# VectorE and ScalarE do the attention's operations between the two parts of an activation step in layer 1, not behind both (Trainium2, one core)

## The chip, the cores and the metric

The kernel runs on one core of a Trainium2 chip, in one launch. The metric is the device time of that launch in microseconds; the kernel before takes 1638.16 us in the median of 3 runs (1637.02 to 1641.31).

## What is computed

```python
a = exp(phi - max_s(phi)); a = a / (sum_s(a) + 1e-9)              # per (batch, head), softmax over the 576 rows
k_m = a^T k;  v_m = a^T v                                         # (32, 64) each: 32 memory slots per head
scores = q k_m^T / 8                                              # (576, 32)
attn = exp(scores - max_m(scores)); attn = attn / (sum_m + 1e-9)
x = attn v_m                                                      # heads side by side: x is (4608, 512)
h = x @ w1_in;  x = where(h > 0, h, exp(min(h, 0)) - 1) @ w1_out  # layer 1: 512 -> 2048 -> 512
h = x @ w2_in;  out = (h * clip(h + 3, 0, 6) / 6) @ w2_out        # layer 2, the same sizes
```

q, k, v and phi are (8, 8, 576, 64) and (8, 8, 576, 32), all float32.

## The kernel before, in words

**Tiling.** Layer 1 works on 16 units of 288 tokens (half a batch entry). A unit has 16 steps `f`, one for each 128 of the 2048 hidden features. In a step TensorE does `up1(f)`, six matmuls of 288 columns into a hidden bank of PSUM (L281 to L283, fed by `pT` and `w`), and `down1(f - 2)`, twelve matmuls that add an earlier step's features into the four accumulators (fed by `g_hi`, `g_lo`). Every product is made in three passes of high and low parts, so each activation leaves as a rounded copy `g_hi` and a rest `g_lo`.

**The step's activation** has five instructions on two engines, `step1`. First part: ScalarE's relu (L499) and exp (L501), then VectorE's combination `g` (L640), which is the last reader of the hidden bank and raises `turn_over`. Second part: ScalarE's copy `g_hi` (L503) and VectorE's `g_lo` (L642). `down1(f)` waits for `g_lo`.

**The attention** of group u + 2 (four heads) is done in the steps of unit u, for u = 0 to 13, as 11 stages; `STEP_OF` gives the step of each: row maximum of phi (S_PHI, step 0), its maximum over partitions (S_MAX, 1), subtraction and exp (S_SUB, 2), k_m and v_m (S_KV, 4), their transposes (S_KMT, 5), transposes of q (S_Q0 and S_Q1, 6 and 7), scores and their subtraction (S_SCORES, 9), exp (S_EXP, 10), sums and reciprocal on VectorE with the product on GpSimd (S_NORM, 11), transposes to `pT` (S_PT, 13). TensorE's instruction of a stage stands behind `up1(f)` and ahead of `down1(f - 2)`.

**Items.** x is never formed: v_m is multiplied into w1_in. That takes 8 items per batch entry: TensorE writes a hidden bank (L352), ScalarE copies `w_hi` (L481), VectorE makes `w_lo` (L633) and raises `turn_over`. Items stand in steps 6, 7, 9, 10, 12, 13 of odd units, 0 and 1 of even ones, and 0 to 3 of unit 0.

**Turns.** `up1` and items use two hidden banks in turn. The one that takes turn t waits until the turns up to t - 2 are over, so `up1` or an item waits for the L640 or L633 two turns back. TensorE's `half` gives the order: `up1(f)`, item, attention stage, `down1(f - 2)`. On ScalarE and VectorE each step was: `step1`, the copies of the last unit's accumulators (`leave`, step 1 only), item, attention stage. Every engine takes its instructions strictly as written, and each `wait_ge` holds all behind it. GpSimd (the product L724, the rests of w_out in unit 0) and SyncE (loads of the next group as soon as stages S_Q1, S_SCORES and S_PT of TensorE are done) are not touched. Layer 2 has no attention.

The few lines that count on VectorE:

```python
dve.wait_ge(e_made, t + 1)
nc.vector.scalar_tensor_tensor(g, g, -1.0, hid(at, HALF), ALU.add, ALU.max).then_inc(turn_over, 1)
dve.wait_ge(g_hi_made, t + 1)
nc.vector.tensor_tensor(g_lo, g, g_hi.bitcast(F32), ALU.subtract).then_inc(g_lo_made, 1)
```

Of the kernel before, what the change touches and what calls it, by code (L numbers as in the profile page):

```python
# [29 lines left out]
def build(nc, q, k, v, phi, w1_in, w1_out, w2_in, w2_out, out):  # L30
# [10 lines left out]
    DC, FC = D // P, F // P  # L41
# [11 lines left out]
    RING = 4  # L53
    AHEAD = 2
# [6 lines left out]
    with ExitStack() as ctx:  # L61
# [14 lines left out]
        def place(name, shape, dt, offset):  # L76
            return nc.alloc_sbuf_tensor_at(name, [P] + shape, dt, offset=base + offset)
# [11 lines left out]
        at = 4 * W  # L89
# [21 lines left out]
        def attention_set(tag, at_kvm, at_rows, at_kv, at_q, bank, stats):  # L111
            t = AttentionSet(bank)
            t.kvm = place("kvm" + tag, [3, P], F32, at_kvm)
            t.kmT = t.kvm[:, 2]
            t.row_max = t.kvm[0:ROWS, 2]
            t.rows = place("rows" + tag, [CH, P], F32, at_rows)


            t.kv = place("kv" + tag, [CH, MAC, KVW], F32, at_kv)
            t.qT = place("qT" + tag, [2, S], F32, at_kv)  # L120
            t.q = [place(f"q{i}" + tag, [CH, 2, DH], F32, x) for i, x in enumerate(at_q)]
            t.stats = stats
            t.phi_loaded, t.kv_loaded = sem("phi_loaded" + tag), sem("kv_loaded" + tag)
            t.q_loaded = [sem(f"q{i}_loaded" + tag) for i in range(2)]
            return t

        A = attention_set("", at, at + 3 * P * 4, a_kv, (a_q0, arena_bytes - Q_BYTES), ATT, small)
# [4 lines left out]
        g1 = [place(f"g1_{i}", [HALF], F32, at + i * ring1) for i in range(2)]  # L132
        g1_hi = place("g1_hi", [RING, HALF], F32R, at + 2 * ring1)
        g1_lo = place("g1_lo", [RING, HALF], F32R, at + (2 + RING) * ring1)
# [49 lines left out]
        def beyond(count):  # L184

            return not isinstance(count, int) or count > 0

        def hid(turn, n):
            return ps[:, HID + turn % 2, 0:n]
# [21 lines left out]
        def halves(a):  # L211
            return a[:].rearrange("p (b c) -> p b c", b=2)
# [4 lines left out]
        def kvm_block(t, h):  # L217
            parity = h % 2
            return t.kvm[h * M:(h + 1) * M, 0:2, parity * DH:(parity + 1) * DH]

        def nth(g, p):

            return 2 * p + g + 1 if isinstance(g, int) and g < AHEAD else 2 * g + p + 1
# [17 lines left out]
        def stages_at(f):  # L241
            return [stage for stage in STAGES if STEP_OF[stage] == f]
# [11 lines left out]
        def item_index(u, parity, n):  # L254
            return 4 * u + n + (NI // 2 if parity else 0)

        def first_turn(u, parity):

            if isinstance(u, int) and u == 0:
                return PRE  # L260
            return 20 * u + (4 if parity else 6)

        def turns(u, parity):

            at, found, made = 0, items_in(u, parity), []
            for f in range(FC):
                n = found.get(f)
                made.append((f, at, n))
                at += 1 if n is None else 2
            return made  # L270
# [181 lines left out]
        def _(act):  # L452
            def attention(g, stage, t, slot):
                if stage == S_SUB:
                    act.wait_ge(a_sub_made, g + 1)
                    nc.scalar.activation(t.rows_flat, t.rows_flat, ACT.Exp).then_inc(a_exp_made, 1)
                elif stage == S_KV:
                    act.wait_ge(a_inv_step, 2 * (g + 1))
                    for h in range(2):
                        rows = slice(h * M, (h + 1) * M)  # L460
                        op = nc.scalar.activation(kvm_block(t, h), t.ps_kv[rows],
                                                  ACT.Copy, scale=t.a_inv[rows])
                    op.then_inc(kv_copied_act, 1)
                elif stage == S_KMT:
                    act.wait_ge(kvT_done, g + 1)
                    nc.scalar.mul(t.kmT, t.ps_kmT, SCALE).then_inc(kmT_copied, 1)
                    nc.scalar.copy(vT[:, slot % 2], t.ps_vT).then_inc(vT_made, 1)
                elif stage in (S_Q0, S_Q1):
                    p = int(stage == S_Q1)
                    act.wait_ge(qT_done, nth(g, p))  # L470
                    nc.scalar.copy(t.qT[:, p, 0:HALF], t.ps_cols[:, 0]).then_inc(q_copied_act, 1)
                elif stage == S_EXP:
                    act.wait_ge(p_sub_step, 2 * (g + 1))
                    nc.scalar.activation(t.rows_flat, t.rows_flat, ACT.Exp).then_inc(p_exp_made, 1)
                elif stage == S_PT:
                    act.wait_ge(pT_done, g + 1)
                    nc.scalar.copy(halves(pT_hi[slot]), t.ps_cols).then_inc(pT_hi_made, 1)

            def item(i, n, at):
                act.wait_ge(item_done, i + 1)  # L480
                nc.scalar.copy(w1_hi[n // 2][:, n % 2], hid(at, BANK)).then_inc(w1_hi_made, 1)  # L481
# [12 lines left out]
            def step1(u, f, at, turn):  # L494
                t = u * FC + f
                if beyond(t - 1):
                    act.wait_ge(g_lo_made, t - 1)
                act.wait_ge(h_done, t + 1)
                nc.scalar.activation(g1[f % 2][:], hid(at, HALF), ACT.Relu, scale=-1.0).then_inc(r_made, 1)  # L499
                act.wait_ge(r_made, t + 1)  # L500
                nc.scalar.activation(g1[f % 2][:], g1[f % 2][:], ACT.Exp, scale=-1.0).then_inc(e_made, 1)  # L501
                act.wait_ge(turn_over, turn + 1)
                nc.scalar.copy(g1_hi[:, f % RING], g1[f % 2][:]).then_inc(g_hi_made, 1)  # L503

# [9 lines left out]
            def leave(u, dst):  # L514
                if beyond(u):
                    act.wait_ge(stored, 16 * u)
                for c in (0, 2):
                    act.wait_ge(acc_done, DC * u + c + 1)
                    nc.scalar.copy(dst[:, c], acc(c, dst.shape[2])).then_inc(acc_copied_act, 1)

            def half(u, um, attend):
                parity, first = um % 2, isinstance(u, int) and u == 0
                last = isinstance(u, int) and u == UNITS1 - 1
                for f, at, n in turns(u, parity):
                    step1(u, f, at, first_turn(u, parity) + at)
                    if f == LAG - 1 and not first:
                        leave(u - 1, y_sb)
                    if n is not None:
                        item(item_index(u, parity, n), n, at + 1)
                    if attend:  # L530
                        for stage in stages_at(f):
                            attention(u + AHEAD, stage, A, (um + AHEAD) % 4)
                    if first:
                        split_out_hi(f, 0)
                    if last:
                        split_in_hi(f)
                        if f >= 10:
                            split_out_hi(f - 10, 1)
# [40 lines left out]
        def _(dve):  # L579
# [55 lines left out]

            def step1(u, f, at):
                t = u * FC + f
                g, g_hi, g_lo = g1[f % 2][:], g1_hi[:, f % RING], g1_lo[:, f % RING]
                dve.wait_ge(e_made, t + 1)
                nc.vector.scalar_tensor_tensor(g, g, -1.0, hid(at, HALF), ALU.add, ALU.max).then_inc(turn_over, 1)  # L640
                dve.wait_ge(g_hi_made, t + 1)
                nc.vector.tensor_tensor(g_lo, g, g_hi.bitcast(F32), ALU.subtract).then_inc(g_lo_made, 1)  # L642

# [19 lines left out]
            def half(u, um, attend):  # L663
                parity, first = um % 2, isinstance(u, int) and u == 0
                for f, at, n in turns(u, parity):
                    step1(u, f, at)
                    if f == LAG - 1 and not first:
                        leave(u - 1, y_sb)
                    if n is not None:
                        item(item_index(u, parity, n), n, at + 1)  # L670
                    if attend:
                        for stage in stages_at(f):
                            attention(u + AHEAD, stage, A, (um + AHEAD) % 4)
                    if isinstance(u, int) and u == UNITS1 - 1 and f == FC // 2:
                        x2_round(0, 0)

# [219 lines left out]
```

## Time and profile before

| what | value |
|---|---|
| median of 3 runs | 1638.16 us (1637.02 to 1641.31) |
| the profiled execution: its own time / its span | 1637.58 us / 1635.8 us |
| mean granted TensorE clock | 0.997 of full speed |
| TensorE busy | 1579.6 us, 97% of the span |
| VectorE, ScalarE, GpSimd busy | 659.4, 654.2, 132.2 us |
| DMA | 79.50 MB, mean 49 GB/s |

The span is from the first to the last instruction; the execution's own time has 1.8 us around it. Matmul rows overlap: consecutive ones start about 0.13 us apart and each is shown for about 0.29 us. "[1.41 <-DVE kvm L583]" behind a row is the idle time of that engine before it and what ended it.

### The profile page before, as it was taken

What the parts mean: (1) busy time and instruction counts of PE and PEld (TensorE: products, weight loads), DVE (VectorE), ACT (ScalarE), POOL (GpSimd) and SP (SyncE); (2) the same over time, 40 slices, a digit from 0 to 9 for tenths busy, and PEclk for the clock granted to TensorE, in tenths of its full rate; (3) what the DMA queues carried; (4) which work ended last, traced back from release to release, by engine and by line L of the source; (5) the groups of instructions that cost most, each with busy time, mean ns of one, the idle gap of its engine ahead of it and who ended that gap; (6) DMA issues with size and microseconds to landing.
All of it is one profiled execution on the core that took longest, in us unless ns stands there. A gap on an engine that the chain in (4) does not pass through costs nothing.

```text
span 1635.8 us, 25445 instructions
## 1 busy us (share of the span) xinstructions
PE 1579.6 (97%) x9840; PEld 1364.1 (83%) x9840; DVE 659.4 (40%) x1163; ACT 654.2 (40%) x1363; POOL 132.2 (8%) x99
## 2 busy tenths in 40 slices
PE   4999999999999999999999999999999999999999
PEld 3788989879888798888998888888888888888887
DVE  4455555554555545555353232232323232323222
ACT  2565555545555455555573222222222222222222
POOL 0320000000000000000182101010101010101000
PEclk9899999999999999999999999999999999999999
DMA  9423221232212222120321010101010101010000
GB/s 246 136 42 66 52 59 42 47 68 52 59 38 52 64 55 59 38 52 17 143 79 65 0 52 0 52 0 51 0 51 0 51 0 51 0 49 2 7 19 26
DMA packets 178101, 79.50 MB, mean 49 GB/s; under 512 B 152400, under 2 KB 160592, under 8 KB 178000
## 3 DMA queue, kind: packets, MB, share of 16 engines
q1 hardware_dynamic: 168528, 76.07, 17.6%
q10 hardware_dynamic: 9472, 2.07, 0.8%
q8 instruction: 65, 1.06, 0.3%
q14 instruction: 36, 0.29, 0.1%
HBM read 59.24 MB, written 18.87 MB: 48 GB/s over the span
## 4 chain that ended last, share of the span: by engine, by line
PE 57%; issue 37%; DVE 2%; ACT 2%; POOL 1%; ACTq 1%; POOLq 0%; DVEq 0%
PE ps L281 18%; PE ps L283 18%; PE ps L282 18%; POOL rows L724 1%; PE ps L352 1%; DVE g L640 1%; PE ps L331 1%; ACT g_hi L503 0%; PE ps L302 0%; ACT g L501 0%; ACT g L499 0%; DVE g_lo L642 0%; ACTq L556 0%; PE ps L320 0%; ACTq L554 0%
## 5 line engine op out<-in xcount | busy, mean ns | idle before, releaser
L281 PE MATMUL ps<-g_hi,w_out_lo 128*128 128x288 f32 x1024 | 314.1, 307 | 0.9 <-POOL w_out_lo L713 0.6
L282 PE MATMUL ps<-g_lo,w_out_hi 128*128 128x288 f32 x1024 | 301.7, 295 | 0.0
L283 PE MATMUL ps<-g_hi,w_out_hi 128*128 128x288 f32 x1024 | 301.7, 295 | 0.0
L509 ACT ACTIVATE g<-ps,one_half 128x512 f32<-128x512 f32 x144 | 99.3, 690 | 465.6 <-PE ps L283 465.6
L648 DVE SCALAR_TENSOR_TENSOR g<-g,ps 128x512 f32<-128x512 f32 x144 | 99.2, 689 | 450.5 <-ACT g L509 450.5
L281 PE MATMUL ps<-x_hi,w_in_lo 128*128 128x512 f32 x576 | 224.1, 389 | 0.0
L283 PE MATMUL ps<-x_hi,w_in_hi 128*128 128x512 f32 x576 | 224.1, 389 | 0.0
L282 PE MATMUL ps<-x_lo,w_in_hi 128*128 128x512 f32 x576 | 224.1, 389 | 0.0
L281 PE MATMUL ps<-w_out_hi,g_lo 128*128 128x512 f32 x576 | 224.1, 389 | 0.0
L282 PE MATMUL ps<-w_out_lo,g_hi 128*128 128x512 f32 x576 | 224.1, 389 | 0.0
L283 PE MATMUL ps<-w_out_hi,g_hi 128*128 128x512 f32 x576 | 224.1, 389 | 0.0
L640 DVE SCALAR_TENSOR_TENSOR g<-g,ps 128x288 f32<-128x288 f32 x256 | 115.4, 451 | 256.8 <-ACT g L501 256.7
L281 PEld LDWEIGHTS ps<-g_hi,w_out_lo 128*128 128x128 f32 x1024 | 192.3, 188 | 23.2 <-issue 20.3
L282 PEld LDWEIGHTS ps<-g_lo,w_out_hi 128*128 128x128 f32 x1024 | 192.5, 188 | 0.1
L283 PEld LDWEIGHTS ps<-g_hi,w_out_hi 128*128 128x128 f32 x1024 | 192.2, 188 | 0.0
L642 DVE TENSOR_TENSOR g_lo<-g,g_hi 128x288 fp32r<-128x288 f32 x256 | 130.5, 510 | 127.8 <-ACT g_hi L503 127.8
L499 ACT ACTIVATE g<-ps 128x288 f32<-128x288 f32 x256 | 104.8, 409 | 179.6 <-PE ps L283 160.7
L503 ACT CAST g_hi<-g 128x288 fp32r<-128x288 f32 x256 | 110.8, 433 | 142.6 <-DVE g L640 142.6
L281 PE MATMUL ps<-pT_hi,w_lo 128*128 128x288 f32 x512 | 151.9, 297 | 4.6 <-issue 3.0
L282 PE MATMUL ps<-pT_lo,w_hi 128*128 128x288 f32 x512 | 151.4, 296 | 0.0
L283 PE MATMUL ps<-pT_hi,w_hi 128*128 128x288 f32 x512 | 151.1, 295 | 0.0
L650 DVE TENSOR_TENSOR g_lo<-g,g_hi 128x512 fp32r<-128x512 f32 x144 | 108.7, 755 | 99.0 <-ACT g_hi L512 99.0
(108 smaller groups left out, 1950.7 us busy)
## 6 DMA issues: line engine op xcount, KB each, us to landing
layer_out<-y_sb SPq DMA_DIRECT2D x16, 576.0 KB, 3.1
x_raw<-layer_out SPq DMA_DIRECT2D x9, 1024.0 KB, 6.9
kv<-in_k SPq DMA_DIRECT2D x60, 144.0 KB, 3.4
kv<-in_v SPq DMA_DIRECT2D x60, 144.0 KB, 3.5
q<-in_q SPq DMA_DIRECT2D x60, 144.0 KB, 2.9
w_in_raw<-in_moe_w_in SPq DMA_DIRECT2D x8, 1024.0 KB, 10.9
w_out_raw<-in_moe_w_out SPq DMA_DIRECT2D x8, 1024.0 KB, 6.2
out<-out_sb SPq DMA_DIRECT2D x8, 1024.0 KB, 5.1
```

The costliest lines, as they stand in the source:

```text
L281: nc.tensor.matmul(dst, a_lo, b_hi, start=first, stop=False)
L282: nc.tensor.matmul(dst, a_hi, b_lo, start=False, stop=False)
L283: return nc.tensor.matmul(dst, a_hi, b_hi, start=False, stop=last)
L331: mm = nc.tensor.matmul(chunk(t, j, P)[0:ROWS, lm], t.qT[:, p, j * ROWS:(j + 1) * ROWS], t.kmT[:, lm], start=True, stop=True)
L352: mm = nc.tensor.matmul(hid(at, BANK)[lm], vT[:, gi, lm], w_in_raw[:, 2 * gi + p, cols], start=True, stop=True)
L499: nc.scalar.activation(g1[f % 2][:], hid(at, HALF), ACT.Relu, scale=-1.0).then_inc(r_made, 1)
L503: nc.scalar.copy(g1_hi[:, f % RING], g1[f % 2][:]).then_inc(g_hi_made, 1)
L509: nc.scalar.activation(g2[f % 2][:], hid(f, BLOCK), ACT.Relu, bias=one_half[:, 0:1], scale=1.0 / 6.0).then_inc(e_made, 1)
L640: nc.vector.scalar_tensor_tensor(g, g, -1.0, hid(at, HALF), ALU.add, ALU.max).then_inc(turn_over, 1)
L642: nc.vector.tensor_tensor(g_lo, g, g_hi.bitcast(F32), ALU.subtract).then_inc(g_lo_made, 1)
L648: nc.vector.scalar_tensor_tensor(g, g, 1.0, hid(f, BLOCK), ALU.min, ALU.mult).then_inc(turn_over, 1)
L650: nc.vector.tensor_tensor(g_lo, g, g_hi.bitcast(F32), ALU.subtract).then_inc(g_lo_made, 1)
```

## The change

In each step of layer 1, ScalarE's and VectorE's part of the attention stage moves from behind the item to between the first part of the activation and the second. The instructions and waits are the same; TensorE's, GpSimd's and SyncE's programs are the same.

```diff
 # ScalarE, step1
                 nc.scalar.activation(g1[f % 2][:], g1[f % 2][:], ACT.Exp, scale=-1.0).then_inc(e_made, 1)
+
+            def step1_hi(u, f, turn):
+
+                t = u * FC + f
                 act.wait_ge(turn_over, turn + 1)
                 nc.scalar.copy(g1_hi[:, f % RING], g1[f % 2][:]).then_inc(g_hi_made, 1)
...
                     step1(u, f, at, first_turn(u, parity) + at)
+                    if attend:
+                        for stage in stages_at(f):
+                            attention(u + AHEAD, stage, A, (um + AHEAD) % 4)
+                    step1_hi(u, f, first_turn(u, parity) + at)
                     if f == LAG - 1 and not first:
                         leave(u - 1, y_sb)
                     if n is not None:
                         item(item_index(u, parity, n), n, at + 1)
-                    if attend:
-                        for stage in stages_at(f):
-                            attention(u + AHEAD, stage, A, (um + AHEAD) % 4)
...
 # VectorE, step1
                 nc.vector.scalar_tensor_tensor(g, g, -1.0, hid(at, HALF), ALU.add, ALU.max).then_inc(turn_over, 1)
+
+            def step1_lo(u, f):
+
+                t = u * FC + f
+                g, g_hi, g_lo = g1[f % 2][:], g1_hi[:, f % RING], g1_lo[:, f % RING]
                 dve.wait_ge(g_hi_made, t + 1)
                 nc.vector.tensor_tensor(g_lo, g, g_hi.bitcast(F32), ALU.subtract).then_inc(g_lo_made, 1)
...
                     step1(u, f, at)
+                    if attend:
+                        for stage in stages_at(f):
+                            attention(u + AHEAD, stage, A, (um + AHEAD) % 4)
+                    step1_lo(u, f)
                     if f == LAG - 1 and not first:
                         leave(u - 1, y_sb)
                     if n is not None:
                         item(item_index(u, parity, n), n, at + 1)
-                    if attend:
-                        for stage in stages_at(f):
-                            attention(u + AHEAD, stage, A, (um + AHEAD) % 4)
```

In the new file the lines of VectorE are five further on: L640 is L645, L642 is L652, L633 is L638, L583 is L588, L612 and L615 are L617 and L620.

VectorE, steps 0 and 1 of an odd unit (S_PHI is the reduction into `kvm`, S_MAX the one of `stats`). Before:

```order
L640 SCALAR_TENSOR_TENSOR g_0_80<-g_0_80,ps 128x288
L642 TENSOR_TENSOR g_lo<-g_0_80,g_hi 128x288
L583 TENSOR_REDUCE kvm<-rows 96x128
L640 SCALAR_TENSOR_TENSOR g_1_81<-g_1_81,ps 128x288
L642 TENSOR_TENSOR g_lo<-g_1_81,g_hi 128x288
L657 COPY y_sb<-ps 128x288 x2
L587 TENSOR_REDUCE stats<-ps 128x1
```

Now:

```order
L645 SCALAR_TENSOR_TENSOR g_0_80<-g_0_80,ps 128x288
L588 TENSOR_REDUCE kvm<-rows 96x128
L652 TENSOR_TENSOR g_lo<-g_0_80,g_hi 128x288
L645 SCALAR_TENSOR_TENSOR g_1_81<-g_1_81,ps 128x288
L592 TENSOR_REDUCE stats<-ps 128x1
L652 TENSOR_TENSOR g_lo<-g_1_81,g_hi 128x288
L667 COPY y_sb<-ps 128x288 x2
```

The two reductions moved ahead of `g_lo`, and the second also ahead of the accumulators' copies.

VectorE, steps 9 and 10 of an odd unit (S_SCORES and an item in step 9, an item in step 10). Before:

```order
L640 SCALAR_TENSOR_TENSOR g_1_81<-g_1_81,ps 128x288
L642 TENSOR_TENSOR g_lo<-g_1_81,g_hi 128x288
L633 TENSOR_TENSOR w_lo_61<-ps,w_hi_57 128x512
L612 TENSOR_REDUCE stats<-ps 96x24
L615 TENSOR_TENSOR rows<-ps,stats 96x768
L640 SCALAR_TENSOR_TENSOR g_0_80<-g_0_80,ps 128x288
```

Now:

```order
L645 SCALAR_TENSOR_TENSOR g_1_81<-g_1_81,ps 128x288
L617 TENSOR_REDUCE stats<-ps 96x24
L620 TENSOR_TENSOR rows<-ps,stats 96x768
L652 TENSOR_TENSOR g_lo<-g_1_81,g_hi 128x288
L638 TENSOR_TENSOR w_lo_61<-ps,w_hi_57 128x512
L645 SCALAR_TENSOR_TENSOR g_0_80<-g_0_80,ps 128x288
```

The item's `w_lo`, which ends a turn, now stands behind the stage's two operations and `g_lo`.

## Rows read from the trace of the kernel before

**Rows 1.** Busy time by engine (PE, PEld, DVE, ACT, POOL) in a stretch of layer 2.

```profile
1000.00:1600.00 600.00, 600.00 (x2649) 496.82 (x2648) 173.71 (x242) 151.74 (x235) 27.68 (x6) 1.00 0.07 23
```

**Rows 2.** Waits of TensorE over the span: us in total, times, longest.

```profile
PE ps L290 <- DVE kvm L583: 18.5, 9, 8.2
PE ps L337 <- POOL rows L724: 8.7, 8, 3.1
PE ps L352 <- DVE w_lo L633: 3.1, 8, 0.7
```

**Rows 3.** Timeline, odd unit, steps 0, 1 and 5: start us, us, instruction, idle before.

```profile
302.91 0.46 DVE L640 SCALAR_TENSOR_TENSOR g<-g,ps 128x288 f32<-128x288 f32 x1 [0.99 <-ACT g L501]
303.86 0.46 DVE L642 TENSOR_TENSOR g_lo<-g,g_hi 128x288 fp32r<-128x288 f32 x1 [0.50 <-ACT g_hi L503]
304.24 1.45 DVE L583 TENSOR_REDUCE kvm<-rows 96x128 f32<-96x768 f32 x1
...
305.74 0.30 PE L290 MATMUL ps<-ident,kvm 96*128 96x96 f32 x1 [1.41 <-DVE kvm L583]
...
215.76 0.14 PEld L308 LDWEIGHTS ps<-ident,kvm 128*128 128x128 f32 x1 [0.25 <-ACT kvm L461]
```

**Rows 4.** Timeline, even unit, steps 0 to 2, VectorE and TensorE.

```profile
254.53 0.45 DVE L640 SCALAR_TENSOR_TENSOR g<-g,ps 128x288 f32<-128x288 f32 x1 [0.97 <-ACT g L501]
...
256.57 1.50 DVE L583 TENSOR_REDUCE kvm<-rows 96x128 f32<-96x768 f32 x1
...
257.07 1.08 PE L352 MATMUL ps<-w_in_raw,vT 128*64 128x512 f32 x4
...
260.58 0.30 PE L283 MATMUL ps<-pT_hi,w_hi 128*128 128x288 f32 x1
261.55 0.35 PE L293 MATMUL ps<-ident,stats 128*96 128x128 f32 x1 [0.67 <-DVE stats L587]
```

**Rows 5.** Timeline, odd unit, items of steps 6, 7, 9 and 10.

```profile
322.91 0.69 DVE L633 TENSOR_TENSOR w_lo<-ps,w_hi 128x512 fp32r<-128x512 f32 x1
...
324.50 1.08 PE L352 MATMUL ps<-w_in_raw,vT 128*64 128x512 f32 x4
...
333.42 0.69 DVE L633 TENSOR_TENSOR w_lo<-ps,w_hi 128x512 fp32r<-128x512 f32 x1
334.26 0.95 DVE L612 TENSOR_REDUCE stats<-ps 96x24 f32<-96x768 f32 x1
335.24 0.95 DVE L615 TENSOR_TENSOR rows<-ps,stats 96x768 f32<-96x768 f32 x1
...
336.60 0.65 PE L352 MATMUL ps<-w_in_raw,vT 128*64 128x512 f32 x2
```

**Rows 6.** Timeline, steps 11 to 13 of an even unit, and the item of step 13 in an odd one.

```profile
292.34 0.39 DVE L640 SCALAR_TENSOR_TENSOR g<-g,ps 128x288 f32<-128x288 f32 x1
293.24 1.06 DVE L642 TENSOR_TENSOR g_lo<-g,g_hi 128x288 fp32r<-128x288 f32 x1 [0.50 <-ACT g_hi L503]
...
292.50 1.48 POOL L724 TENSOR_TENSOR rows<-rows,stats 96x768 f32<-96x768 f32 x1 [48.74 <-DVE stats L625]
...
294.04 0.38 PE L337 MATMUL ps<-ident,rows 96*128 96x96 f32 x2 [0.73 <-POOL rows L724]
...
346.57 0.65 PE L352 MATMUL ps<-w_in_raw,vT 128*64 128x512 f32 x2 [0.32 <-DVE w_lo L633]
```

**Rows 7.** Timeline, unit 0, steps 2 and 3: VectorE's subtraction, TensorE's item.

```profile
56.30 0.94 DVE L590 TENSOR_TENSOR rows<-rows,ps 96x768 f32<-96x768 f32 x1
...
57.56 0.65 PE L352 MATMUL ps<-w_in_raw,vT 128*64 128x512 f32 x2
```

**Rows 8.** Groups of ScalarE over the span: busy us, mean ns of one, idle before.

```profile
L503 ACT CAST g_hi<-g 128x288 fp32r<-128x288 f32 x256 | 110.8, 433 | 142.6 <-DVE g L640 142.6
L481 ACT CAST w_hi<-ps 128x512 fp32r<-128x512 f32 x64 | 37.1, 582 | 1.0 <-PE ps L352 0.9
L456 ACT ACTIVATE rows<-rows 96x768 f32<-96x768 f32 x15 | 12.7, 846 | 19.6 <-DVE rows L590 19.6
```

More of the change, by code:

```diff
@@ L637, in step1 @@
                 t = u * FC + f
-                g, g_hi, g_lo = g1[f % 2][:], g1_hi[:, f % RING], g1_lo[:, f % RING]
+                g = g1[f % 2][:]
                 dve.wait_ge(e_made, t + 1)
                 nc.vector.scalar_tensor_tensor(g, g, -1.0, hid(at, HALF), ALU.add, ALU.max).then_inc(turn_over, 1)
+            def step1_lo(u, f):
+                t = u * FC + f
+                g, g_hi, g_lo = g1[f % 2][:], g1_hi[:, f % RING], g1_lo[:, f % RING]
                 dve.wait_ge(g_hi_made, t + 1)
```

## The prediction, made before the changed kernel was run

> **What bounds the kernel now.** I read the busy time by stretch first. In layer 2 TensorE has no gap at all: 600.00 us busy in a stretch of 600.00 [rows 1]. So nothing on the other engines can be won there, and whatever TensorE gains or loses in layer 1 arrives whole at the end of the kernel. Then I read the waits of TensorE [rows 2]. They are short and belong to the attention: it waits for VectorE's row maximum at L290 (9 times; one of 8.2 us is in the start-up, 7 are the 1.41 us of the odd units), for GpSimd's product at L337, and for the `w_lo` of an item at L352. Each is a place where the attention's work is ready later than TensorE is. Last, the timeline of one even and one odd unit, step by step, because the change only reorders two engines inside a step: the question at each step is what stands in front now, what stands behind, and how long TensorE can do without it.
>
> The pattern that the change uses is in [rows 3]: VectorE finishes `g` at 303.37, then idles 0.50 us until ScalarE has copied `g_hi`, makes `g_lo` from 303.86, and only then starts the reduction at 304.24 (instructions without a wait start 0.08 us before the one ahead is shown ended). With the stage in between, its VectorE operation starts 0.95 us earlier (304.24 less 303.29) if its input is there, and part of it fills that idle time. In return `g_lo`, and behind it an item's `w_lo`, are later.
>
> **Odd units (1, 3, ... 13: seven).**
> - L290, step 1. The reduction ends at 303.29 + 1.45 = 304.74 and TensorE goes on 0.05 us later as before, at 304.79 for 305.74 [rows 3]. **-0.95 us**, all of it inside the wait of 1.41.
> - L308, step 5, waits 0.25 us for the copies of k_m and v_m [rows 3]; those copies also start about 1 us earlier against TensorE. **-0.2 us**.
> - Step 6. `w_lo` is now behind the copy of q: ScalarE's copy waits for TensorE's transposes, so I get `w_lo` ending at 324.16, for 323.60 before. The next item needs it at 324.50 [rows 5]. Hidden, with 0.34 us left of a cover of 0.90; if that cover fell short the price would be the rest.
> - Step 9, the expensive one. L612 cannot start earlier: it waits for TensorE's scores, at 334.26 either way. L612 and L615 end at 336.19; then come `g_lo` (336.11 to 336.57) and `w_lo` (336.59 to 337.28), which used to end at 334.11. The item of step 10 needs that bank at 336.60 [rows 5] and starts at 337.33. **+0.73 us**, a wait that does not exist now.
> - Step 11 to 13. The item of step 13 waits 0.32 us for `w_lo` [rows 6], because the `g_lo` ahead in the queue takes 1.06 us instead of 0.46 while GpSimd's L724 runs. In the new order the sums, the reciprocal and then `g_lo` of step 11 follow each other, and GpSimd's product is triggered earlier relative to TensorE, which step 10 has held back 0.73. I get this `w_lo` ready before TensorE comes: **-0.32 us**.
>
> Together -0.95 - 0.2 + 0.73 - 0.32 = -0.74, times 7: **-5.2 us**.
>
> **Even units (2, 4, ... 12: six).**
> - Step 0. The reduction runs from 254.90 to 256.40, `g_lo` to 256.78, `w_lo` to 257.49; the item of step 1 starts at 257.54 for 257.07 [rows 4]. **+0.47 us**.
> - Step 2. L293 waits 0.67 us for the maximum L587, which stands behind the copies of the accumulators and an item's `w_lo` [rows 4]. In the new order it stands ahead of them. TensorE could start L293 at 260.58 + 0.15 and, with the 0.47 from above, does at 261.20 for 261.55. **-0.82 us**, net of step 0 -0.35.
> - Steps 11 to 13. L724 is triggered 0.95 us earlier. The row says who comes first: the VectorE instruction behind the reciprocal starts at 292.34, GpSimd at 292.50 [rows 6], so the new follower `g_lo` is ahead of GpSimd by 0.16 us. That `g_lo` and L724 disturb each other is seen from the other side: `g_lo` takes 1.06, ending 0.32 after L724. If GpSimd waits for `g_lo`, it starts 0.38 later, at 291.93, ends at 293.41, and L337 starts at 293.47 for 294.04: **-0.57 us**. Without such a wait it would be up to the whole 0.73 idle. I take the first.
>
> The Trainium skill (SBUF — State Buffer, section "Who interferes with whom") says that a VectorE operation with two SBUF inputs and a GpSimd operation that reads SBUF exclude each other for a whole instruction, the first to start keeping the ports. The row with 1.06 us agrees with its half "the loser fully blocks"; no row shows VectorE starting first. By that rule the term is the one taken; by the other reading of the row, sharing without order, it would be up to -0.73 and the sum 1 us lower.
>
> Together -0.92, times 6: **-5.5 us**.
>
> **Unit 0** has items in steps 0 to 3 beside stages 0 to 2, and a loss. In step 2, `w_lo` moves from ahead of L590 (56.30) to behind L590 (0.94), ScalarE's exp (0.85), `g_hi` (0.43), `w_hi` (0.58) and its own 0.69 [rows 7, 8]. L590 itself starts about 1 us earlier, at some 55.5; the chain of 3.5 us ends near 59.0 where the item of step 3 started at 57.56: +1.5. A phi load that lands late in step 0 can add 1; the earlier product in step 11 gives back about 0.65. I take **+1.5 us**; bounds 0 and +2.5.
>
> **What else moves.** A later `g_lo` is needed by `down1` and by relu two steps on. The largest delay, in step 9, leaves it ready at 336.57, before even the item of step 10 begins, and its users are in step 11: nothing; without that cover it would cost what exceeds it. No stage waits for something of its own step that now stands behind it. SyncE's loads follow TensorE and have their own queue: not delayed. Units 14 and 15 and layer 2: zero.
>
> **The sum.** -5.2 - 5.5 + 1.5 = -9.2 us against the profiled execution's 1637.58: 1628.4. The median shown is 0.6 higher, so **1629 us**, -0.56%. A measurement of this kernel can tell a change over 0.3%, about 4.9 us, from none: below 1633.2 counts as faster.
>
> **Rivals.**
> - **B, GpSimd comes first in step 11.** Then `g_lo` of step 11 is held until 0.32 after L724, and g, `g_hi`, `w_hi`, `w_lo` of step 12 queue behind it. I get `w_lo` at 347.78 for an item that started at 346.57 [rows 6]: odd units -1.15 + 1.26 = +0.11, six even ones -0.35 - 0.87 (L337 no longer waits at all): 0.8 - 7.3 + 1.5 = -5.0, **1633**. For it: 0.16 us is a thin lead. Against: in-order start after the reciprocal without any wait. The Trainium skill (SBUF — State Buffer, the same section) makes the start decide, so a swap of 0.16 us would bring exactly this case.
> - **C, the odd units give everything back.** TensorE comes to the items earlier, but they are paced by the two other engines, whose chain of turns is longer now. For it: they wait at L352 already [rows 2]. Against: those engines are triggered by TensorE's own matmuls, which come earlier too. Odd units 0, even -5.5, unit 0 +1.5: -4.0, **1634**, not to be told from no change.
> - **D, slower.** One mechanism: each late `w_lo` of an odd unit reaches TensorE in full, as it would if an item had to wait for the turn right before its own, or if the covers at L352 were not there: 0.56 (step 6) + 3.17 (step 9) + 1.26 (step 12) = 5.0 per odd unit, less 1.15: +3.85, times 7 is 27; with -5.5 + 1.5, +23: **1661**. It decides as soon as the items' waits of an odd unit exceed about 1.7 us, for I have 0.41 of them. Against: covers of 0.90 and 2.49 us are in [rows 5].
> - **E**, the good end: the scores' operations start in time and no wait at step 10 arises: -0.73 times 7, **1624**.
>
> **How the numbers follow.** Forecast 0.62 (with E in it), B 0.16, C 0.14, D 0.08. Faster: 0.62 and some two thirds of B, which stands on the border: 0.72. Same: C and the rest of B, 0.20. Slower: D, 0.08. The range goes from a little below E, 1622, to beyond B and C with the upper bound of unit 0, 1636.
>
> **What the changed profile would show.** Right: L290's wait down to about 0.5 us in odd units; a new wait of about 0.7 us of TensorE at L352 for `w_lo` in step 10; L293's wait gone; L337's wait under 0.2; `g_lo` of step 11 at 0.46 us and GpSimd starting behind it. Wrong: `g_lo` of step 11 lasting over 1 us (B), waits at L352 of more than 1.5 us per odd unit (C, D), or a wait of `down1` for `g_lo` anywhere, which I have at nothing.

## The result, and the profile after

The changed kernel takes 1621.39 us in the median of 4 runs (1619.87 to 1622.8), for 1637.68 (1637.02 to 1641.31) of the kernel before: a ratio of 0.9898, 95% interval 0.9884 to 0.9911, 16.3 us less. It is faster, as forecast, but by 16 us where 9 were forecast, and it lies 0.6 us below the range. The profiled execution took 1620.48 us, its span is 1618.8 (1635.8 before). The ratios, here and below, are estimated over all executions, so they need not equal the quotient of the two medians (here 0.9901). One execution of the kernel before, among those beside runs 5, 7 and 8, took 4019 us and is left out of the ratios.

TensorE's waits after the change, to be read beside [rows 2] (us in total, times, longest; each line number of VectorE is five up, of GpSimd eleven):

```profile
PE ps L290 <- DVE kvm L588: 11.8, 8, 8.2
...
PE ps L352 <- DVE w_lo L638: 9.2, 16, 1.2
PE ps L337 <- POOL rows L735: 3.1, 1, 3.1
```

One line of the kernel before is gone without a successor:

```profile
PE ps L293 <- DVE stats L587: 4.0, 6, 0.7
```

L290's wait fell by 6.7 us. L337 kept only the 3.1 us of the start-up: in the units it is gone altogether. L352 rose from 3.1 us to 9.2.

Step 1 of the odd unit, timeline, beside [rows 3]. The reduction starts 0.08 us before `g` is shown ended, and `g_lo` follows without an idle time:

```profile
298.10 0.45 DVE L645 SCALAR_TENSOR_TENSOR g<-g,ps 128x288 f32<-128x288 f32 x1 [0.99 <-ACT g L501]
298.47 1.51 DVE L588 TENSOR_REDUCE kvm<-rows 96x128 f32<-96x768 f32 x1
299.89 0.45 DVE L652 TENSOR_TENSOR g_lo<-g,g_hi 128x288 fp32r<-128x288 f32 x1
...
300.03 0.30 PE L290 MATMUL ps<-ident,kvm 96*128 96x96 f32 x1 [0.52 <-DVE kvm L588]
```

Steps 9 and 10 of the odd unit, timeline, beside [rows 5]: the scores' two operations, `g_lo` and `w_lo` now stand in one row, and the item waits for the last of them:

```profile
328.17 0.95 DVE L617 TENSOR_REDUCE stats<-ps 96x24 f32<-96x768 f32 x1 [1.82 <-PE ps L331]
329.16 0.95 DVE L620 TENSOR_TENSOR rows<-ps,stats 96x768 f32<-96x768 f32 x1
330.03 0.45 DVE L652 TENSOR_TENSOR g_lo<-g,g_hi 128x288 fp32r<-128x288 f32 x1
330.39 0.68 DVE L638 TENSOR_TENSOR w_lo<-ps,w_hi 128x512 fp32r<-128x512 f32 x1
...
331.13 0.65 PE L352 MATMUL ps<-w_in_raw,vT 128*64 128x512 f32 x2 [0.55 <-DVE w_lo L638]
```

Steps 11 to 13 of the even unit, timeline, beside [rows 6]:

```profile
287.21 0.30 DVE L630 RECIPROCAL stats<-stats 96x24 f32<-96x24 f32 x1
287.43 0.39 DVE L652 TENSOR_TENSOR g_lo<-g,g_hi 128x288 fp32r<-128x288 f32 x1
288.04 0.45 DVE L645 SCALAR_TENSOR_TENSOR g<-g,ps 128x288 f32<-128x288 f32 x1 [0.22 <-ACT g L501]
288.99 0.48 DVE L652 TENSOR_TENSOR g_lo<-g,g_hi 128x288 fp32r<-128x288 f32 x1 [0.50 <-ACT g_hi L507]
...
287.59 1.57 POOL L735 TENSOR_TENSOR rows<-rows,stats 96x768 f32<-96x768 f32 x1 [47.44 <-DVE stats L630]
...
289.16 0.29 PE L283 MATMUL ps<-pT_hi,w_hi 128*128 128x288 f32 x1
289.29 0.33 PE L337 MATMUL ps<-ident,rows 96*128 96x96 f32 x2
```

`g_lo` is first, GpSimd starts at its usual distance of 0.08 us behind the reciprocal and lasts 1.57 us instead of 1.48. TensorE goes from `up1(13)` into L337 at once, 0.13 us after the last matmul.

**A ledger.** TensorE has the same instructions in the same order in both kernels. So its start times can be subtracted, instruction by instruction, and each step in the difference is one wait that went or came (or, as run 2 shows, a stretch at another clock). Per unit, from one L337 to the next, and beside the forecast's terms (us):

| | forecast | measured |
|---|---|---|
| odd: L290 | -0.95 | -0.95 |
| odd: L293 and L302 | 0 | -0.16 |
| odd: L308 | -0.20 | -0.21 |
| odd: item of step 10 | +0.73 | +0.62 |
| odd: item of step 13 | -0.32 | -0.40 |
| **odd, sum, times 7** | -0.74, -5.2 | -1.12, **-7.8** |
| even: item of step 1 | +0.47 | +0.39 |
| even: L293, from there | -0.82 | -0.90 |
| even: L302 and steps 6 to 9 | 0 | -0.20 |
| even: L337 | -0.57 | -0.90 |
| **even, sum, times 6** | -0.92, -5.5 | -1.66, **-9.9** |
| **unit 0** | +1.5 | **-0.5** |
| **layer 1** | -9.2 | **-18.3** |

(The row of L290 has 0.90 us at L290 itself and 0.05 at L337's matmuls ahead of it. The rows of an odd unit make -1.10 and those of an even one -1.61; the means over all units have some hundredths more.) Behind layer 1 nothing changes: the difference at the last matmul of the program is the one at the last item, within 0.02 us, in this profile and in the eleven others of the study. The spans differ by 17.0, not by 18.3, since up to the first matmul of unit 0 the second profile is 1.2 us longer. That part is looked at below.

### The profile page after: what moved, and what is told of

It reads as the page before. It is cut to its first block, busy times and chain, and to the rows that moved or that the text cites. A ratio compares the mean times of both kernels' runs of the same rounds, so it can differ in the third digit from the quotient of the medians.

```text
span 1618.8 us, 25445 instructions
## 1 busy us (share of the span) xinstructions
PE 1572.7 (97%) x9840; PEld 1364.0 (84%) x9840; DVE 650.2 (40%) x1163; ACT 650.4 (40%) x1363; POOL 133.5 (8%) x99
## 3 DMA queue, kind: packets, MB, share of 16 engines
q1 hardware_dynamic: 168528, 76.07, 17.8%
q8 instruction: 65, 1.06, 0.3%
## 4 chain that ended last, share of the span: by engine, by line
PE 90%; DVE 4%; ACT 3%; issue 2%; ACTq 1%; POOL 0%; DVEq 0%
PE ps L281 27%; PE ps L283 27%; PE ps L282 27%; PE ps L352 3%; PE ps L331 2%; PE ps L302 2%; PE ps L320 1%; DVE kvm L588 1%; ACT g L501 1%; DVE g_lo L652 1%; ACT g L499 1%; DVE g L645 1%; DVE w_lo L638 1%; PE ps L337 1%; ACT g_hi L507 0%
## 5 line engine op out<-in xcount | busy, mean ns | idle before, releaser
L645 DVE SCALAR_TENSOR_TENSOR g<-g,ps 128x288 f32<-128x288 f32 x256 | 116.2, 454 | 247.3 <-ACT g L501 246.4
L652 DVE TENSOR_TENSOR g_lo<-g,g_hi 128x288 fp32r<-128x288 f32 x256 | 119.3, 466 | 99.1 <-ACT g_hi L507 97.2
```

## The experiments

The kernels of the study take the changed kernel and let a condition say which stages stand early; the others stand where they stood before:

```diff
                     step1(u, f, at)
                     if attend:
-                        for stage in stages_at(f):
+                        for stage in (x for x in stages_at(f) if early(first, parity, x)):
                             attention(u + AHEAD, stage, A, (um + AHEAD) % 4)
                     step1_lo(u, f)
...
                         item(item_index(u, parity, n), n, at + 1)
+                    if attend:
+                        for stage in (x for x in stages_at(f) if not early(first, parity, x)):
+                            attention(u + AHEAD, stage, A, (um + AHEAD) % 4)
```

and the same on ScalarE. "Layer 1" below is the difference to the first profile of the kernel before between the first item of unit 0 and the last item, by TensorE's start times.

**1. The first two stages alone** (`early`: `stage in (S_PHI, S_MAX)`).

> Only the row maximum and its maximum over partitions (stages S_PHI and S_MAX, steps 0 and 1) stand early. Theory by ledger (each wait of TensorE moves the end by itself, terms add): seven odd units gain 0.95 us at L290 and 0.1 at L293, six even ones lose 0.4 at the item of step 1 and gain 0.85 at L293; unit 0 about +0.4: near 10 us less than the kernel before, 1627 to 1629 us. Rival (the gains of one stage are taken back at the items of steps 6 to 13, or come from something all stages share): under 5 us less, over 1632.5.

1632.63 us, ratio 0.9954 (0.9937 to 0.9972) to a kernel before of 1641.01 on that chip; layer 1 shorter by 7.6 us. Odd units -0.91, even ones -0.21. L290 and L293 gave about what the theory says (-0.90 and -0.16; +0.39 and -0.90). But part is given back one wait later: the copies of k_m and v_m in step 4 are now late for L308. The weight load shows it in an odd unit, where it waited 0.25 us before [rows 3]:

```profile
318.25 0.14 PEld L314 LDWEIGHTS ps<-ident,kvm 128*128 128x128 f32 x1 [0.41 <-ACT kvm L467]
```

So the terms stand, and a wait that was hidden behind them came up: 0.15 us in odd units, 0.38 in even ones. Expected were 10 us, measured 7.6 to 8.4, neither what the theory said nor the rival's under 5.

**2. The first four** (`stage in (S_PHI, S_MAX, S_SUB, S_KV)`).

> Stages of steps 0 to 4 early (S_PHI, S_MAX, S_SUB, S_KV). With S_PHI and S_MAX alone layer 1 was 7.6 us shorter, 5 less than their terms in the changed kernel, since the copies of k_m and v_m of step 4 were late for L308 (0.15 us in odd, 0.37 in even units). Ledger: with S_KV early too these are won back: layer 1 shorter by 12 to 13, unit 0 then costs its 1.2 of step 2: about 11.5 us less than the kernel before. Rival (stages add with no such link): 8 to 9 less.

1631.15 us, 0.9947 (0.9932 to 0.9963); layer 1 shorter by 10.0. Even units -0.61, unit 0 +1.24; six of the seven odd units -1.30, but unit 1 +0.17. The link is there: with S_KV early the even units and those six odd ones win back 0.40 each. What sets unit 1 apart is TensorE's clock. From 96.2 to 99.6 us of this profile the granted clock is 0.50, the lower of its two levels (1.2 GHz), and matmuls start 0.24 us apart instead of 0.13:

```profile
96.30:99.50 3.20, 3.20 (x15) 3.20 (x15) 1.64 (x3) 1.49 (x3) 2.38 (x2) 0.50 0.57 90
```

```profile
96.96 0.45 PE L288 MATMUL ps<-g_lo,w_out_hi 128*128 128x288 f32 x1
97.20 0.45 PE L289 MATMUL ps<-g_hi,w_out_hi 128*128 128x288 f32 x1
```

That costs 1.54 us. Without it layer 1 would be shorter by some 11.6 us (10.0 + 1.54), beside the 11.5 that were expected. The four executions of this kernel have mean granted clocks of 0.993 to 0.996, those of the kernel before on that chip 0.995 to 0.998, so its times probably hold such a stretch too. Why the clock fell here stays open: TensorE is busy for 4.27 of the 6.00 us ahead of it in this profile, and for 4.27 of 6.00 in the same place of the kernel before, where it did not fall.

**3. The sums alone** (`stage == S_NORM`).

> Only the sums and the reciprocal (S_NORM, step 11, VectorE) stand early. Ledger from the changed kernel's trace (GpSimd starts 0.95 us earlier and is held up by 0.1 us at most): even units -0.9 at L337, odd ones -0.4 at L352 of step 13, unit 0 about -1: near 9 us less, 1628 to 1630. Rival, the prediction's term (GpSimd waits 0.38 us for g_lo): even -0.57, odd -0.32, unit 0 -0.65: 6.3 less, 1631.4.

1630.21 us, 0.9935 (0.9918 to 0.9951); layer 1 shorter by 9.0: even units -0.90 each, odd ones -0.39, unit 0 -0.86. This one stage, three operations on VectorE, makes half of the whole gain, and the prediction's smaller term for it is refuted. `g_lo` is ahead of GpSimd here too (even unit):

```profile
292.74 0.39 DVE L661 TENSOR_TENSOR g_lo<-g,g_hi 128x288 fp32r<-128x288 f32 x1
292.90 1.57 POOL L747 TENSOR_TENSOR rows<-rows,stats 96x768 f32<-96x768 f32 x1 [48.26 <-DVE stats L639]
```

**4. The scores alone** (`stage == S_SCORES`).

> Only the scores' maximum and subtraction (S_SCORES, step 9, VectorE) stand early. Ledger: a new wait of 0.6 to 0.75 us of TensorE at the item of step 10 in each of seven odd units and nothing gained anywhere: 4.3 to 5.1 us more, 1642 to 1643. Rival (the wait is only time that the item of step 13 would wait anyway, 0.32 us): 2 to 3 more, 1640.

1645.56 us, 1.0035 (1.0023 to 1.0048); layer 1 longer by 4.2, 0.63 in each odd unit, at the item of step 10 and nowhere else. Slower, as the ledger said: this part of the change is a loss by itself.

**5. The other stages** (`stage not in (S_PHI, S_MAX, S_SCORES, S_NORM)`).

> All stages but S_PHI, S_MAX, S_SCORES and S_NORM early. TensorE waits almost nowhere for these: L308 in odd units (0.2, seven times) and 0.1 per even unit; unit 0 pays 1.2 in step 2. Layer 1 shorter by 0.5 to 1.5 us, time the same. Rival (ScalarE's earlier exps and copies are worth something by themselves): over 4 us less.

1636.61 us, 0.9988 (0.9978 to 0.9997); layer 1 shorter by 3.0, twice what I had expected at most: 0.26 in each unit on average, unit 0 longer by 0.4. In the odd units nearly all of it is L308 (0.21 to 0.24); in the even ones it is spread over steps 6 to 9 (0.14) and L337 (0.10). The rival with over 4 us fell.

**6. VectorE alone** (ScalarE as before).

> VectorE as in the changed kernel, ScalarE as in the kernel before. Theory (all waits of TensorE that shrank end at VectorE or at GpSimd, which VectorE triggers; ScalarE's part only fills its own idle time): within 3 us of the changed kernel, 1621 to 1624. Rival (ScalarE's earlier copies and exps carry a good part): over 1627.

1623.49 us, 0.9893 (0.9876 to 0.9909), not to be told from the whole change; layer 1 shorter by 17.8, of 18.3. ScalarE's half of the edit is worth half a microsecond of layer 1, and that is a balance: it gains about 1.0 us over units 1 to 13 and loses 0.5 in unit 0, where without it the item of step 3 is not late.

**7. Unit 0 alone** (`first`).

> The new order in unit 0 alone. Prediction's term: 1.5 us more. Ledger of the changed kernel: the item of step 3 1.2 us later and that of step 1 0.4, taken back by clock and overlap in steps 1 and 2 (0.6) and by L337 (1.2 to 1.5): unit 0 0.4 to 0.5 us shorter, time the same as before within noise.

1641.0 us, 1.0012 (1.0002 to 1.0022); layer 1 shorter by 0.4 us. By the two medians (1639.13 for the kernel before) the times and the ledger disagree by some 2 us, which stays open. Beside the ten executions of run 8, again the kernel before, it is only 0.8 us more, and of the two profiles this one has the shorter span (1639.1 for 1639.4). The start-up of this profile is 3.7 us longer than that of the first one, which is the next run's subject. TensorE's row at the item of step 3 shows the loss that was forecast: 62.46 for 57.56 before [rows 7], of which 3.67 are the start-up and 1.2 the wait:

```profile
62.46 1.08 PE L358 MATMUL ps<-w_in_raw,vT 128*64 128x512 f32 x4 [1.18 <-DVE w_lo L647]
```

Up to L337 of this unit 1.6 us come back, 1.34 of them at L337, so it ends 0.4 shorter. The item of step 1 is 0.36 us late as well, but `up1(2)` behind it starts where it did, 6.9 us after the unit's first matmul. It had waited for the `g` of step 1 anyway, and the granted clock rises from 0.50 to full just there: the item's first matmul takes 0.61 us for 0.80 in run 8's profile.

**8. The kernel before, again.**

> The kernel before once more, for its profile: the 46 us up to the first matmul of unit 0 came out 0.5 to 4.4 us longer in the profiles of all other kernels than in the first profile of the kernel before. If that is chance of the start-up's loads, this profile shows it too (1 to 5 us longer up to that matmul) and layer 1 behind it equal within 0.2 us. If it is the order's doing, the start-up is as short as in the first profile.

1640.2 us, ratio 1.0001 (0.9991 to 1.0011). Layer 1 is the same to 0.01 us and its units within some hundredths, but for two even ones that differ by 0.20 and 0.23 the opposite way. The start-up is not the same: the first matmul of unit 0 stands at 45.13 us in the first profile and at 48.69 in this one, with the same program:

```profile
48.69 0.58 PE L281 MATMUL ps<-pT_hi,w_lo 128*128 128x288 f32 x1 [1.61 <-DVE pT_lo L628]
```

Their first matmuls at L302 are level (20.52 and 20.54 us); the profiles part between 24 and 34.6 us, where the same instructions of TensorE take up to 1.7 times as long. First profile:

```profile
26.76 0.69 PE L320 MATMUL ps<-ident,q 96*128 96x96 f32 x6
29.21 1.94 PE L352 MATMUL ps<-w_in_raw,vT 128*64 128x512 f32 x8
```

This one:

```profile
27.70 1.16 PE L320 MATMUL ps<-ident,q 96*128 96x96 f32 x6
31.68 3.03 PE L352 MATMUL ps<-w_in_raw,vT 128*64 128x512 f32 x8
```

So it is TensorE at its lower rate for 10 us longer, though the column of the granted clock reads 1.00 there. Over the eleven profiles of the other runs and the changed kernel the first matmul of unit 0 came between 0.5 and 4.4 us later than in the first one: six of them have the long slow stretch and come 3.6 us or more later, the other five 0.5 to 1.6. Up to 1.3 us more is there before the stretch (the first matmul at L302, L308 in most runs, stands at 20.5 to 21.8 us). Since one program gave both, it is chance, worth up to 4 us in a time, and no part of the change. The ledger of layer 1 leaves it out; the times can't.

**9. The changed kernel, again.**

> The changed kernel once more, beside the others of this call on one chip: 16 to 18 us under the kernel before. The first 46 us, up to the first matmul of unit 0, may differ by some us from profile to profile without any change in the order there; layer 1 behind it should again be 18.3 us shorter than in the profile of the kernel before.

1623.38 us beside 1639.02: 0.9901 (0.9886 to 0.9916). Layer 1 shorter by 18.27, for 18.31 in the first profile of this kernel, though the start-up is 3.2 us longer than there.

**10. Two operations ahead of GpSimd.**

```diff
+                if attend and f == STEP_OF[S_NORM]:
+                    nc.vector.tensor_tensor(spare[:], g, g_hi.bitcast(F32), ALU.subtract)
                 nc.vector.tensor_tensor(g_lo, g, g_hi.bitcast(F32), ALU.subtract).then_inc(g_lo_made, 1)
```

> The changed kernel with one more subtraction of 128x288 from two SBUF tensors (into a spare tile) ahead of g_lo in step 11: VectorE has two of them running when GpSimd's L735 is triggered. Theory of a first-come lock for a whole instruction: L735 gets the ports after the first one (about 0.1 us late) and the second, the real g_lo, lasts until 0.3 us after L735, 1.5 to 1.9 us. Rival (VectorE wins as long as it has such work, or both share): the second lasts 0.5 to 0.9 us and L735 is 0.4 us longer or more. Time: 1 to 8 us over the changed kernel, by what queues behind g_lo in odd units.

1625.28 us, 0.9914 (0.9899 to 0.9929), 1.9 over the changed kernel beside it; layer 1 is 4.9 us longer than with the change. Some 2.5 of these belong to the added operation (0.29 at L337 in each even unit, 0.36 in unit 0, 0.05 per odd unit). The other 2.4 are the late phi load that the prediction feared in unit 0:

```profile
50.94 1.50 DVE L598 TENSOR_REDUCE kvm<-rows 96x128 f32<-96x768 f32 x1 [0.97 <-DMA rows<-in_phi]
```

It holds `w_lo` and the item of step 1 back (TensorE is idle for 2.57 us before it), and at the end of that wait the granted clock falls to 0.50, for 3.4 us. Timeline of step 11, even unit:

```profile
290.79 0.30 DVE L640 RECIPROCAL stats<-stats 96x24 f32<-96x24 f32 x1
291.01 0.39 DVE L663 TENSOR_TENSOR spare<-g,g_hi 128x288 f32<-128x288 f32 x1
291.32 0.44 DVE L664 TENSOR_TENSOR g_lo<-g,g_hi 128x288 fp32r<-128x288 f32 x1
...
292.62 0.80 DVE L664 TENSOR_TENSOR g_lo<-g,g_hi 128x288 fp32r<-128x288 f32 x1 [0.50 <-ACT g_hi L514]
...
291.17 1.94 POOL L750 TENSOR_TENSOR rows<-rows,stats 96x768 f32<-96x768 f32 x1 [47.07 <-DVE stats L640]
```

The rival is right in the main (0.44 us for its 0.5 to 0.9, and 0.46 longer for its 0.4 or more). GpSimd's operation is shown from 291.17, yet the second VectorE operation starts after it, at 291.32, and is not held up; GpSimd lasts 1.94 us, 0.46 longer than the 1.48 of the kernel before. All 14 units show the same numbers to 0.01 us. In the kernel before, an operation stands in the very place of the first one, 0.16 us ahead of GpSimd and 0.39 long, but it reads `g` from SBUF and the other input from PSUM (L640, [rows 6]), and GpSimd lasts its 1.48. That points to the second input from SBUF, though the two operations differ in kind too. The `g_lo` of the next step, which comes while GpSimd really runs, lasts 0.80 and ends 0.31 after it. Whether GpSimd stands still for those 0.46 us or runs slowly, these rows don't tell. Nor do they tell when it asks for its first input: the 0.23 and 0.59 us that VectorE still has to do at GpSimd's shown start cost it 0.09 and 0.46, both some 0.13 less, and by that estimate it asks at 291.30, almost level with the second operation's start.

**11. A version without the losses.** `early` is true but for S_SCORES of odd units, S_PHI of even units and of unit 0, and S_SUB of unit 0.

> The changed order but for three places, where a wait at L352 appeared: S_SCORES of odd units, S_PHI of even units and of unit 0, and S_SUB of unit 0 stand where they stood before. Ledger: the new waits at the item of step 10 (0.62, seven times), at the item of step 1 (0.4, six times) and in unit 0 (1.2 and 0.4) go, the gains stay: 7 to 8.5 us less than the changed kernel. Rival (TensorE then waits at the next place for something that these waits covered): under 4 us less.

1613.07 us (1612.48 to 1615.08), 0.9844 (0.983 to 0.9857) to the kernel before and 10.3 us under the changed kernel on the same chip. Layer 1 is shorter by 25.2 us, 6.9 more than with the change, a little under the 7 to 8.5 that were expected: 4.4 in the odd units, 1.6 in the even ones (0.26 each, for 0.4), 0.9 in unit 0 (for 1.6). The start-up, 3.9 us shorter in this profile than in that of run 9, would account for the rest. The waits at L352 (here L358) are nearly all gone; of the others only L290's (here L296) grew, from 11.8 us to 12.8:

```profile
PE ps L296 <- DVE kvm L597: 12.8, 10, 8.1
...
PE ps L343 <- POOL rows L747: 3.1, 1, 3.1
...
PE ps L358 <- DVE w_lo L647: 1.3, 2, 0.7
```

## Why the prediction was too low

The direction and the mechanism were right. TensorE bounds the kernel, what it waits for in layer 1 is the attention's part on VectorE and GpSimd, and in units 1 to 13 each wait won or lost adds up unit by unit and arrives at the end undiminished, unless the next stage's result then comes late (L308 in run 1). Rival C, that the odd units give all back, is out, since they keep 1.12 us each. L290, L308, L293 and the three places of L352 are within 0.11 us of their terms. Rival D is out too: the items of an odd unit wait 0.62 us in all. Sizes were off, all to the same side, and the steps that failed are these:

- **L337 and GpSimd, "it starts 0.38 later, at 291.93": 0.33 us too little, times 6, 2 us.** That `g_lo` comes first was right, and rival B is out. But I let GpSimd wait for all of `g_lo`. `g_lo` is 0.16 us ahead and lasts 0.39, and L735 took only 0.09 longer, in all 14 units: it pays for less than the 0.23 that `g_lo` still has to do. Run 10, with twice the work ahead, makes it 0.46 us longer, and L337 waits again. With 0.09 L735 is done 0.13 us before TensorE comes, so L337's wait goes altogether, which is the 0.87 that I had put under rival B.
- **"What else moves ... nothing": 0.16 us per odd and 0.20 per even unit missing, 2.3 us.** I had looked only for a wait that would be added. Around L293, L302, L320 and L331 TensorE had lost 0.04 to 0.09 us each that the list of its waits does not show; those went. Run 1 shows the 0.16 of an odd unit and 0.07 of an even one, run 5 the other 0.14 of an even one.
- **Unit 0, "I take +1.5": it is -0.5, 2 us.** The term's core was right, 1.24 us at the item of step 3. The late phi load did not come in this profile (it did in run 10's): the item of step 1 starts only 0.45 later, and nothing of that arrives at `up1(2)`. L337 and the last `down1` ahead of it give back 1.46 for the 0.65 that I had.
- The rest are small errors of one sign: 0.62 for 0.73 and 0.40 for 0.32 in odd units (1.3 us over seven), 0.39 for 0.47 and 0.90 for 0.82 in even ones (1.0 over six), and some hundredths per unit. The idle time that the profile shows before a matmul is 0.07 to 0.16 short of what the start times give (0.32 for 0.39 at the item of step 13, 0.73 for 0.89 at L337), because the matmul ahead is still shown as running; I had taken 0.32 from the row.

Together these are 9 us in layer 1; the start-up's chance, 1.2 us between the two profiles, goes against them. My bounds had the same fault: they let the losses be larger in unit 0 and at L352, and the only good end was a missing wait at step 10, at the full price of a term. That L337 might gain its whole wait stood in the text and was not carried into the lower end of the range: 6 times 0.3 would have taken it to 1620.

The even units and GpSimd: the Trainium skill (SBUF — State Buffer, section "Who interferes with whom") says that the first to start keeps the shared ports for its instruction. The changed kernel's trace agrees (`g_lo` first, 0.39 us, GpSimd 0.09 longer). Run 10 does not, if "start" is the start in the profile: GpSimd's was shown 0.15 us ahead of the second VectorE operation, and lost. If it is the moment in which GpSimd asks, estimated above at 291.30, the two are too close to tell.

## What to carry to other kernels

When two orders of the same instructions are compared, subtract the start times of the engine that bounds, instruction by instruction: one profile of each gives every wait that went or came, to 0.1 us, and layer 1 repeated to 0.04 us where times scatter by 3. Look at the granted clock of both profiles first: two of the thirteen have a further stretch of 3.4 us at 0.50 behind the first steps of unit 0, and in run 2 it made 1.5 us that no wait explains. Work that is put into the idle time between two dependent operations is paid by what stands behind the second: here it gained wherever TensorE waited for the stage's result, and lost where the stage's input came late (the scores) or an item's bank had to be freed behind it. Move stage by stage, not all at once; the same edit with three stages partly left where they were shortened layer 1 by 25.2 us instead of 18.3.

## What was not expected of the hardware

- Two back-to-back operations of VectorE on two SBUF tensors each lost nothing themselves (0.39 and 0.44 us) and made GpSimd's 0.46 us longer (1.94 for 1.48), although GpSimd's was shown starting before the second. The other way round VectorE's waits until GpSimd is done: 1.06 us for 0.46 [rows 6] and 0.80 in run 10, each ending 0.31 to 0.32 us after GpSimd.
- The same program took 45.1 or 48.7 us up to the same matmul, because TensorE ran at its lower rate until about 34 us instead of 24 (run 8). What decides that, and why the clock fell in unit 1 of run 2, was not tried.
